# Merged input loads, four buffers of third weights and three of raw weights in the weight stage

## The chip, the cores and the metric

The kernel runs on one core of a Trainium2 chip. The metric is the time of the whole program on the device in microseconds, the median of the runs. A core has TensorE (PE in the profile), VectorE (DVE), ScalarE (ACT), GpSimd (POOL) and SyncE (SP); SP issues nearly all DMA transfers of this kernel.

## The reference, cut to what matters

```python
# attention with a decaying state, B, H, S, D = 4, 8, 768, 48
for t in range(S):
    cur = einsum('bhd,bhe->bhde', u[None] * kt, vt)
    y[:, :, t] = einsum('bhd,bhde->bhe', rt, state + cur)
    state = wt[:, :, :, None] * state + einsum('bhd,bhe->bhde', kt, vt)
# first feed-forward, x is y as [3072, 384], d_ff = 1024
h = ((x @ w1) * (x @ w2)) @ w3
x = h @ w_out
# second: gates choose two of 8 experts per token, then relu(x @ w1[e]) @ w2[e], weighted
```

## The kernel before

Attention goes batch by batch (4), and in a batch by pairs of heads (4). A pair is called g here, from 0 on, over all batches. One head of the pair lies on partitions 0 to 47, the other on 64 to 111. A pair needs the transposed w, k and r (tiles `wt`, `kt`, `rt`, [128, 768]), the rows of k and r (`kn`, `rn`) and of v (`vs`), each in two buffers by the parity of the pair.

The stage that this case is about is the first, some 106 us long. It threads two strands into one order, which every engine follows by itself (the list `order`):

- The attention of batch 0. For pair g the steps are "derive" (DVE: `dve_decays` L254, three reciprocals L265, `dve_keys` L272, `dve_queries` L278), "diag" (DVE: products L289 and L295, the sum L304), "spread" (ACT L317), "score" (PE L186, then the mask on DVE L325, in two halves), "keys" (PE transposes L195, ACT L245), "state" (PE L207, ACT L341, DVE L335), "scale" (ACT L353) and "out" (PE L231 and L237, ACT L360). The derive, diag and spread steps of pair g + 1 stand between the steps of pair g.
- The weights. `w_out` is turned and multiplied with the gates (L658, L667, L674), and then w3 @ w_out is built in eight blocks of rows, q = 0 to 7 ("w3_mm", four quarters each, PE L682). Block q reads `w3T[q % 2]`. ACT rounds the sum to `wah` (L598), and DVE takes the rest `wal` (L623). Beside it the six blocks of w1 and w2 come through `wraw` (two buffers) and are split into `w12h` (ACT L595, after the second quarter of blocks 1 to 6) and `w12l` (DVE L638).

Before its loop SP issues the loads of pairs 0 and 1, of w_out, of w3 blocks 0 and 1 (L526) and of raw blocks 0 and 1 (L532). In the loop, at the last quarter of block q, it asks for w3 block q + 2, once block q is done (`wa_full`), and for raw block q + 1, once `w12l_ready` has reached q. At the derive and diag steps of pair g it asks for the inputs of pair g + 2, at "out" it stores y and asks for v. The loads of pair 2 are the first that the loop issues, ahead of anything else.

`sp_input_load` loads w, k or r of a pair in two transfers, one for each head: 64 rows each for pairs 0 and 1 (which fills the pad rows once), 48 rows each from pair 2 on.

After this stage the feed-forward of batch b runs threaded with the attention of batch b + 1, then the experts. The first thing of it is L788 on PE, which needs the rounded y (`xh`, `xl`) of batch 0.

Of the kernel before, what the change touches and what calls it, by code (L numbers as in the profile page):

```python
# [7 lines left out]
F1 = 1024  # L8
E, F2 = 8, 1024
N = B * S  # L10
P = 128
# [21 lines left out]


TAIL = 3

WORDS = 16
PADS = 14
# [19 lines left out]
def program(nc, w_turned, k_turned, r_turned, k_rows, r_rows, v_rows, u, w1, w2, w3_turned, w_out, gate_rows, noise_rows, ew1, ew2_rows, out):  # L58
# [10 lines left out]
    with top:  # L69
# [70 lines left out]

        def sp_input_load(sp, b, q, n):
            g, i = HP * b + q, q % 2
            rows = HB if g < 2 else D
            need(sp, (decay_ready, kdiv_ready, rdec_ready)[n], g - 1)
            for h in range(2):
                sp.dma_start((wt, kt, rt)[n][i][h * HB:h * HB + rows, :],
                             (w_turned, k_turned, r_turned)[n][bass.ds(b, 1), 2 * q + h, 0:rows, :].rearrange("o d t -> (o d) t")
                             ).then_inc(loaded[n][i], 16)

        def sp_rows_load(sp, b, q):  # L150
            g, i = HP * b + q, q % 2
# [96 lines left out]
        def dve_decays(dve, b, q):  # L248

            g = HP * b + q  # L250
            dve.wait_ge(loaded[0][q % 2], 32 * (2 * b + q // 2 + 1))
            need(dve, state_ready, (NC - 1) * (g - 1))
            for c in range(NC):
                last = nc.vector.tensor_tensor_scan(decay[q % 2][:, c, 1:C + 1], wt[q % 2][:, c * C:(c + 1) * C],  # L254
                                                    wt[q % 2][:, c * C:(c + 1) * C], 1.0, ALU.mult, ALU.bypass)
            last.then_inc(decay_ready, 1)
# [10 lines left out]

        def dve_keys(dve, b, q):
            g = HP * b + q
            dve.wait_ge(loaded[1][q % 2], 32 * (2 * b + q // 2 + 1))  # L270
            dve.wait_ge(inverse_ready, 3 * (g + 1))
            nc.vector.tensor_tensor(kdiv[q % 2][:, :], kt[q % 2][:, :], kdiv[q % 2][:, :], ALU.mult).then_inc(kdiv_ready, 1)  # L272

        def dve_queries(dve, b, q):
            g = HP * b + q
            dve.wait_ge(loaded[2][q % 2], 32 * (2 * b + q // 2 + 1))
# [220 lines left out]

        with ExitStack() as ph:
            psb, psem = tools(ph)
            wraw = [psb(f"wraw{i}", [P, F1]) for i in range(2)]  # L500
            wo = psb("wo", [P, KF, WA])
            gates = psb("gates", [P, KD, 4 * E])
            woT = nc.alloc_sbuf_tensor_at("woT", [P, KD, F1], f32, offset=token_base)
            gates_side = nc.alloc_sbuf_tensor_at("gates_side", [P, 2 * P], f32, offset=token_base + 4 * KD * F1)
            w3T = [psb(f"w3T{i}", [P, KF, P]) for i in range(2)]
            pads = psb("pads", [P, PADS, WORDS], i32)
            wraw_loaded = [sem(f"wraw_loaded{i}") for i in range(2)]
            w12h_ready, w12l_ready = sem("w12h_ready"), sem("w12l_ready")
            wo_loaded, gates_loaded, w3_loaded = [sem(f"wo_loaded{i}") for i in range(2)], sem("gates_loaded"), [sem(f"w3_loaded{i}") for i in range(2)]
# [12 lines left out]

            def first_sp(sp):
                def load_w3(n):
                    need(sp, wa_full, n - 1)
                    sp.dma_start(w3T[n % 2][:, :, :].rearrange("p m j -> p (m j)"), w3_turned[n, :, :]).then_inc(w3_loaded[n % 2], 16)  # L526

                def load_w12(n):
                    m, kk = divmod(n, KD)
                    if n >= 2:  # L530
                        sp.wait_ge(w12l_ready, n - 1)
                    sp.dma_start(wraw[n % 2][:, :], (w1, w2)[m][kk * P:(kk + 1) * P, :]).then_inc(wraw_loaded[n % 2], 16)  # L532
# [12 lines left out]
                sp_values_load(sp, 0, 0)  # L545
                load_w3(1)
                for n in range(3):
                    sp_input_load(sp, 0, 1, n)
                sp_rows_load(sp, 0, 1)
                load_w12(0)  # L550
                sp_values_load(sp, 0, 1)
                load_w12(1)
                for step, q, n in order:
                    if step == "w3_mm" and n == 3:
                        if q + 2 < KF:
                            load_w3(q + 2)
                        if 1 <= q < 2 * KD - 1:
                            load_w12(q + 1)
                    elif step == "derive" or step == "diag":
                        sp_attention(sp, 0, step, q, n)  # L560
                    elif step == "out":
                        sp_attention(sp, 0, step, q, n)
                        if (q, n) == (1, 0):
                            sp.wait_ge(pads_ready, 1)
                            sp.dma_start(slot_entry.rearrange("(p a n) o -> p a (n o)", p=P, a=PADS),
                                         pads[:, :, :].rearrange("p n o -> p (n o)").rearrange("p (a x) -> p a x", a=1)
                                         .broadcast_to([P, PADS, PADS * WORDS])).then_inc(pads_stored, 16)
                            sp.wait_ge(zeros_ready, 1)
                            sp.dma_start(x2[N:N + 1, :].rearrange("o (h d) -> o h d", h=2),
                                         zeros[0:1, :].rearrange("p (h d) -> p h d", h=1).broadcast_to([1, 2, DM // 2])).then_inc(row_cleared, 16)  # L570
                        if (q, n) == (HP - 1, 1):
                            sp_group_load(sp, 0, 0, 1)
                    elif (step, q, n) == ("score", HP - 1, 1):
                        sp_group_load(sp, 0, 0, 0)

            def first_act(act):
# [7 lines left out]
                for step, q, n in order:  # L584
# [3 lines left out]
                    elif step == "wo_gates":  # L588
                        act.wait_ge(gates_full, 1)
                        nc.scalar.copy(gates_side[:, :], fx[:, 0:2 * P]).then_inc(gates_out, 1)  # L590
                    elif step == "w3_mm" and n == 1 and 1 <= q <= 2 * KD:

                        m, kk = divmod(q - 1, KD)
                        act.wait_ge(wraw_loaded[(q - 1) % 2], 16 * ((q - 1) // 2 + 1))
                        nc.scalar.copy(w12h[:, m, kk, :], wraw[(q - 1) % 2][:, :]).then_inc(w12h_ready, 1)  # L595
# [20 lines left out]
            def first_dve(dve):  # L616
# [10 lines left out]
                for step, q, n in order:  # L627
# [6 lines left out]
                    elif step == "w3_mm" and n == 2 and 1 <= q <= 2 * KD:  # L634

                        m, kk = divmod(q - 1, KD)
                        dve.wait_ge(w12h_ready, q)
                        nc.vector.tensor_tensor(w12l[:, m, kk, :], wraw[(q - 1) % 2][:, :], w12h[:, m, kk, :].bitcast(f32),  # L638
                                                ALU.subtract).then_inc(w12l_ready, 1)
                    elif step == "w3_mm" and n == 0 and q:  # L640
                        low(q - 1)
# [4 lines left out]
            def first_pe(pe):  # L646
                pe.wait_ge(ident_ready, 1)
                pe.wait_ge(pad_zero, 2)
                for step, q, n in order:
# [25 lines left out]
                        last.then_inc(gates_full, 1)  # L675
                    elif step == "w3_mm":
                        if n == 0:
                            pe.wait_ge(w3_loaded[q % 2], 16 * (q // 2 + 1))
                            pe.wait_ge(wo_ready, 1)
                            need(pe, wal_ready, q - 1)  # L680
                        for m in range(2 * n, 2 * n + 2):
                            last = nc.tensor.matmul(sums[q % 2][:, 0:WA], w3T[q % 2][:, m, :], wo[:, m, :],  # L682
                                                    start=(m == 0), stop=(m == KF - 1))
                        if n == 3:
                            last.then_inc(wa_full, 1)
# [998 lines left out]
def laid_out(np, inputs):  # L1684
# [1 line left out]
    a = {name: np.asarray(x) for name, x in inputs.items()}  # L1686

    def turned(x, fill):
        return np.pad(x.transpose(0, 1, 3, 2), [(0, 0), (0, 0), (0, HB - D), (0, 0)], constant_values=fill)

    def rows(x, pad):
        x = x.reshape(B, HP, 2, NC, P, D).transpose(0, 1, 4, 3, 2, 5)
# [30 lines left out]
```

## Time and profile before

| | us |
|---|---|
| median of 3 runs | 997.93 (997.01 to 1000.2) |
| the profiled execution, its time | 993.22 |
| its span, first to last instruction | 991.5 |
| PE busy in the span | 951.2 (96%) |
| DVE busy | 676.3 (68%) |
| ACT busy | 528.1 (53%) |

The profiled execution was 4.7 us shorter than the median of the runs; 1.7 us of its time lie outside the span. The span is that of one core, so there is no other core to wait for.

### The profile page before, as it was taken

What the parts mean: (1) busy time and instruction counts of PE and PEld (TensorE: products, weight loads), DVE (VectorE), ACT (ScalarE), POOL (GpSimd) and SP (SyncE); (2) the same over time, 40 slices, a digit from 0 to 9 for tenths busy, and PEclk for the clock granted to TensorE, in tenths of its full rate; (3) what the DMA queues carried; (4) which work ended last, traced back from release to release, by engine and by line L of the source; (5) the groups of instructions that cost most, each with busy time, mean ns of one, the idle gap of its engine ahead of it and who ended that gap; (6) DMA issues with size and microseconds to landing.
All of it is one profiled execution on the core that took longest, in us unless ns stands there. A gap on an engine that the chain in (4) does not pass through costs nothing.

```text
span 991.5 us, 18086 instructions
## 1 busy us (share of the span) xinstructions
PE 951.2 (96%) x6825; PEld 895.8 (90%) x6825; DVE 676.3 (68%) x1133; ACT 528.1 (53%) x986; POOL 221.3 (22%) x209
## 2 busy tenths in 40 slices
PE   5799999999999999999989999999999999999995
PEld 3455899999999999999989999999999999999995
DVE  5688886969696966256766685656856558566570
ACT  3354454555454645325644575655756557565560
POOL 0000000020202020221443323344232432324311
PEclk9889999999999999999999999999999999999998
DMA  9968434353435121216548797877968779787751
GB/s 262 295 190 263 142 85 143 105 160 95 143 106 172 57 71 41 81 52 217 177 123 244 196 294 214 241 257 205 308 206 243 262 202 301 211 245 258 212 152 17
DMA packets 93771, 179.61 MB, mean 181 GB/s; under 512 B 19042, under 2 KB 50532, under 8 KB 93684
## 3 DMA queue, kind: packets, MB, share of 16 engines
q1 hardware_dynamic: 80308, 157.77, 50.7%
q0 software_dynamic: 12976, 20.66, 10.1%
q8 instruction: 54, 0.88, 0.4%
q14 instruction: 33, 0.27, 0.1%
q10 hardware_dynamic: 400, 0.02, 0.0%
HBM read 152.81 MB, written 26.97 MB: 181 GB/s over the span
## 4 chain that ended last, share of the span: by engine, by line
PE 86%; DVE 3%; DMA 3%; ACT 2%; SPq 2%; issue 2%; another core or an unknown queue 0%; POOL 0%; DVEq 0%; ACTq 0%; POOLq 0%
PE pp L1233 20%; PE bank L1217 19%; PE bank L788 13%; PE bank L805 7%; PE fx L788 6%; PE fx L805 4%; PE yu L1276 3%; PE pp L186 2%; DMA w3T<-in_moe_w 2%; PE tr L1198 2%; PE yu L1258 1%; PE fx L1258 1%; PE yu L207 1%; PE yu L237 1%; DMA rn<-in_r_rows 1%
## 5 line engine op out<-in xcount | busy, mean ns | idle before, releaser
L1127 POOL DMA_INDIRECT result<-x2s,who x55 | 92.4, 1681 | 292.5 <-ACT x2s L1350 279.6
L1337 DVE SCALAR_TENSOR_TENSOR abl<-bank,abh 128x512 fp32r<-128x512 f32 x96 | 66.2, 691 | 113.7 <-ACT abh L1332 90.0
L978 POOL DMA_INDIRECT slot_entry<-entry,slot_i x48 | 52.1, 1086 | 334.6 <-DVE token_f L967 322.4
L1217 PE MATMUL bank<-xh,set_up_h 128*128 128x256 f32 x384 | 109.2, 284 | 0.0
L1217 PE MATMUL bank<-xh,set_up_l 128*128 128x256 f32 x384 | 108.6, 283 | 0.0
L1217 PE MATMUL bank<-xl,set_up_h 128*128 128x256 f32 x384 | 108.6, 283 | 0.0
L1332 ACT ACTIVATE abh<-bank 128x512 fp32r<-128x512 f32 x96 | 57.5, 599 | 85.1 <-PE bank L1217 80.2
L788 PE MATMUL bank<-xh,w12h 128*128 128x384 f32 x264 | 89.5, 339 | 1.0 <-DVE xl L485 0.9
L788 PE MATMUL bank<-xh,w12l 128*128 128x384 f32 x264 | 88.4, 335 | 0.0
L788 PE MATMUL bank<-xl,w12h 128*128 128x384 f32 x264 | 88.2, 334 | 0.0
L1233 PE MATMUL pp<-set_down_h,abh 128*128 128x384 f32 x256 | 87.7, 342 | 0.0
L1233 PE MATMUL pp<-set_down_h,abl 128*128 128x384 f32 x256 | 85.7, 335 | 0.0
L1233 PE MATMUL pp<-set_down_l,abh 128*128 128x384 f32 x256 | 85.6, 334 | 0.0
L265 DVE RECIPROCAL kdiv<-decay 128x256 f32<-128x256 f32 x48 | 82.2, 1734 | 0.3
L1114 POOL DMA_INDIRECT tokens<-ffn_out,who x55 | 72.6, 1319 | 32.9 <-issue 23.3
L1217 PEld LDWEIGHTS bank<-xh,set_up_h 128*128 128x128 f32 x384 | 73.5, 191 | 0.5 <-DVE abl L1337 0.2
L1217 PEld LDWEIGHTS bank<-xl,set_up_h 128*128 128x128 f32 x384 | 73.5, 192 | 0.3
L1217 PEld LDWEIGHTS bank<-xh,set_up_l 128*128 128x128 f32 x384 | 73.5, 191 | 0.0
L1350 ACT ACTIVATE x2s<-pp,who 128x384 f32<-128x384 f32 x48 | 28.0, 582 | 84.3 <-PE pp L1233 75.5
L317 ACT ACTIVATE att<-ident,diag 128x128 f32<-128x128 f32 x192 | 59.4, 389 | 15.0 <-DVE diag L304 15.0
L1305 DVE TENSOR_TENSOR set_up_l<-up_raw,set_up_h 128x1024 fp32r<-128x1024 f32 x48 | 57.6, 1224 | 9.3 <-ACT set_up_h L1300 8.8
L1305 DVE TENSOR_TENSOR w12l<-up_raw,w12h 128x1024 fp32r<-128x1024 f32 x45 | 55.0, 1223 | 8.5 <-ACT w12h L1300 5.6
(254 smaller groups left out, 2646.2 us busy)
## 6 DMA issues: line engine op xcount, KB each, us to landing
up_raw<-in_moe_w SPq DMA_DIRECT2D x93, 512.0 KB
down_raw<-in_moe_w SPq DMA_DIRECT2D x124, 384.0 KB
vs<-in_v_rows SPq DMA_DIRECT2D x16, 384.0 KB, 3.6
kn<-in_k_rows SPq DMA_DIRECT2D x16, 288.0 KB, 3.6
rn<-in_r_rows SPq DMA_DIRECT2D x16, 288.0 KB, 4.8
attention_out<-yt SPq DMA_DIRECT2D x64, 72.0 KB, 2.0
result<-zeros SPq DMA_DIRECT2D x12, 384.0 KB
ffn_out<-x2s SPq DMA_DIRECT2D x8, 576.0 KB
```

Of the source, the lines that this page charges most:

```text
L265: nc.vector.reciprocal(kdiv[q % 2][:, :].rearrange("p (c x) -> p c x", c=NC)[:, two, :], decay[q % 2][:, two, 1:C + 1]).then_inc(inverse_r ...
L317: last = nc.scalar.activation(att[:, j, h, c, :], ident[:, :], ACT.Copy, scale=diag[:, 3 * j + c, h:h + 1])
L788: last = nc.tensor.matmul(half_bank[n % 3][:, 0:TG], wp[:, m, kk, f * P:(f + 1) * P], xp[:, kk, :], start=(p == 0), stop=(p == 3 * KD - 1))
L805: last = nc.tensor.matmul(sum_at[s][:, 0:WA], xp[:, f, s * P:(s + 1) * P], wp[:, f, :], start=(f == 0 and n == 0), stop=(f == KF - 1 and n ...
L978: nc.gpsimd.indirect_dma_start(slot_entry, bass.IndirectOffsetOnAxis(slot_i[:, s, n:n + 1], 0), entry[:, s, n, :], None).then_inc(scattere ...
L1114: nc.gpsimd.indirect_dma_start(xg[v % 2][:, s, :], None, stored, bass.IndirectOffsetOnAxis(who[v % 4][:, s, 0:1], 0)).then_inc(gathered[v ...
L1127: nc.gpsimd.indirect_dma_start(out, bass.IndirectOffsetOnAxis(who[v % 4][:, s, 0:1], 0), yo[v % 2][:, s, 0:DM], None, bounds_check=N - 1, ...
L1217: last = nc.tensor.matmul(bank[m % 2][:, f * T2:(f + 1) * T2], wp[:, kk, c:c + P], xp[:, kk, :], start=(n == 0), stop=(n == 3 * KD - 1))
L1233: last = nc.tensor.matmul(pp[:, s, 0:DM], xp[:, f, s * P:(s + 1) * P], wp[:, f, :], start=(f == 0 and n == 0), stop=(f == KF - 1 and n == 2))
L1305: nc.vector.tensor_tensor(low, src, high.bitcast(f32), ALU.subtract).then_inc(w_low, 1)
L1332: nc.scalar.activation(hh[:, 2 * m:2 * m + 2, :].rearrange("p a t -> p (a t)"), bank[m % 2][:, :], ACT.Relu).then_inc(hh_ready, 1)
L1337: nc.vector.scalar_tensor_tensor(hl[:, 2 * m:2 * m + 2, :].rearrange("p a t -> p (a t)"), bank[m % 2][:, :], 0.0, hh[:, 2 * m:2 * m + 2, : ...
```

## The change

Two edits. (1) The arrays w, k and r are laid out in memory as [B, 4, 128, S], the two heads of a pair behind each other with the pad rows in them, so that one transfer of 128 partitions (384 KB) takes the place of two of 64 or 48 (192 or 144 KB each); the waits count 16 instead of 32. (2) `w3T` has four buffers instead of two, `wraw` three instead of two. Before the loop w3 blocks 2 and 3 and raw block 2 are asked for too; in the loop block q + 4 and raw block q + 2. What each of these loads waits for in the loop is unchanged (block q done; `w12l_ready` at q), it only fetches a later block.

```diff
+DEEP, RAW = 4, 3
         def sp_input_load(sp, b, q, n):
-            rows = HB if g < 2 else D
             need(sp, (decay_ready, kdiv_ready, rdec_ready)[n], g - 1)
-            for h in range(2):
-                sp.dma_start((wt, kt, rt)[n][i][h * HB:h * HB + rows, :],
-                             (w_turned, k_turned, r_turned)[n][bass.ds(b, 1), 2 * q + h, 0:rows, :].rearrange("o d t -> (o d) t")
-                             ).then_inc(loaded[n][i], 16)
+            sp.dma_start((wt, kt, rt)[n][i][:, :],
+                         (w_turned, k_turned, r_turned)[n][bass.ds(b, 1), q, :, :].rearrange("o x t -> (o x) t")
+                         ).then_inc(loaded[n][i], 16)
...
-            wraw = [psb(f"wraw{i}", [P, F1]) for i in range(2)]
+            wraw = [psb(f"wraw{i}", [P, F1]) for i in range(RAW)]
-            w3T = [psb(f"w3T{i}", [P, KF, P]) for i in range(2)]
+            w3T = [psb(f"w3T{i}", [P, KF, P]) for i in range(DEEP)]
...
                 def load_w3(n):
-                    need(sp, wa_full, n - 1)
+                    need(sp, wa_full, n - DEEP + 1)
...
                 def load_w12(n):
-                    if n >= 2:
-                        sp.wait_ge(w12l_ready, n - 1)
+                    need(sp, w12l_ready, n - RAW + 1)
...
                 load_w12(0)
                 sp_values_load(sp, 0, 1)
+                load_w3(2)
                 load_w12(1)
+                load_w3(3)
+                load_w12(2)
                 for step, q, n in order:
                     if step == "w3_mm" and n == 3:
-                        if q + 2 < KF:
-                            load_w3(q + 2)
-                        if 1 <= q < 2 * KD - 1:
-                            load_w12(q + 1)
+                        if q + DEEP < KF:
+                            load_w3(q + DEEP)
+                        if 1 <= q <= 2 * KD - RAW:
+                            load_w12(q + RAW - 1)
```

## Rows read from the trace of the kernel before

**Rows 1.** Page, part 2, granted TensorE clock in 40 equal slices.

```profile
...
PEclk9889999999999999999999999999999999999998
...
```

**Rows 2.** Busy time by stretch; last the clock, the DMA share and GB/s.

```profile
...
core 0: us, PE busy (x) PEld busy (x) DVE busy (x) ACT busy (x) POOL busy (x), PEclk, DMA share, GB/s
0.00:49.50 49.50, 30.32 (x198) 18.87 (x200) 29.14 (x43) 18.36 (x45) 1.72 (x13) 0.93 1.00 279
...
60.00:92.00 32.00, 28.66 (x201) 17.53 (x199) 27.90 (x41) 18.49 (x48) 0.00 (x0) 1.00 0.94 287
...
106.00:360.00 254.00, 254.00 (x2046) 239.71 (x2048) 205.50 (x420) 127.41 (x336) 26.12 (x24) 1.00 0.41 121
...
```

**Rows 3.** Timeline of PE: start, duration; idle time before it in brackets.

```profile
...
46.31 3.04 PE L682 MATMUL fx<-wo,w3T 128*128 128x400 f32 x4 [6.05 <-DMA w3T<-in_moe_w]
49.28 1.66 PE L186 MATMUL pp<-rdec,kdiv 48*128 48x128 f32 x12
50.86 1.31 PE L207 MATMUL yu<-vs,kend_t 128*64 128x48 f32 x20
...
59.15 1.61 PE L682 MATMUL fx<-wo,w3T 128*128 128x400 f32 x4
...
65.42 0.94 PE L186 MATMUL pp<-rdec,kdiv 48*128 48x128 f32 x12 [0.63 <-issue]
...
69.20 0.79 PE L207 MATMUL yu<-vs,kend_t 128*64 128x48 f32 x20
71.34 2.95 PE L682 MATMUL fx<-wo,w3T 128*128 128x400 f32 x8 [1.36 <-DMA w3T<-in_moe_w]
...
80.80 4.30 PE L682 MATMUL bank<-wo,w3T 128*128 128x400 f32 x12 [1.35 <-DMA w3T<-in_moe_w]
85.03 0.94 PE L186 MATMUL pp<-rdec,kdiv 48*128 48x128 f32 x12
...
```

**Rows 4.** Busy time by stretch around the longest wait.

```profile
...
42.00:46.00 4.00, 0.00 (x0) 0.00 (x0) 0.00 (x0) 0.00 (x0) 0.00 (x0) 0.54 1.05 251
...
50.00:56.00 6.00, 6.00 (x36) 3.97 (x33) 4.26 (x12) 2.84 (x7) 0.00 (x0) 0.50 0.05 20
56.00:60.00 4.00, 4.00 (x50) 2.68 (x49) 4.00 (x4) 0.96 (x2) 0.00 (x0) 1.00 0.25 74
...
```

**Rows 5.** Timeline of DVE, the same columns.

```profile
...
40.58 0.74 DVE L289 TENSOR_TENSOR ruk<-kn,rn 128x576 f32<-128x576 f32 x1
41.24 0.57 DVE L623 TENSOR_TENSOR wal<-bank,wah 128x400 fp32r<-128x400 f32 x1
51.05 1.01 DVE L325 COPY_PREDICATED att<-causal,pp 128x768 f32<-128x768 int32 x1 [9.24 <-PE pp L186]
...
53.70 2.00 DVE L254 TENSOR_TENSOR_SCAN decay<-wt 128x128 f32<-128x128 f32 x6
...
82.66 0.95 DVE L278 TENSOR_TENSOR rdec<-rt,decay 128x768 f32<-128x768 f32 x1
...
86.08 1.02 DVE L325 COPY_PREDICATED att<-causal,pp 128x768 f32<-128x768 int32 x1 [1.28 <-PE pp L186]
...
```

**Rows 6.** The chain that ended the first stage: start, duration, what.

```profile
...
7.79 10.19 DMA rn<-in_r_rows
...
```

**Rows 7.** Stretches of the first 40 us; the last column is GB/s.

```profile
...
2.75:5.50 2.75, 0.00 (x0) 0.00 (x0) 0.01 (x1) 0.01 (x1) 0.00 (x0) 1.00 1.00 233
...
8.00:13.80 5.80, 4.07 (x18) 3.48 (x19) 4.50 (x3) 1.81 (x4) 0.00 (x0) 1.00 1.07 262
...
19.00:25.00 6.00, 4.60 (x45) 3.20 (x47) 3.12 (x5) 4.40 (x14) 0.00 (x0) 1.00 1.03 241
25.00:28.00 3.00, 3.00 (x25) 1.78 (x20) 2.46 (x9) 1.91 (x6) 0.00 (x0) 1.00 1.04 357
31.00:38.50 7.50, 6.53 (x20) 3.41 (x18) 7.36 (x9) 4.64 (x14) 0.00 (x0) 1.00 1.04 232
...
```

**Rows 8.** Tile rn, the transfer of pair 2, issued at 22.21.

```profile
...
DMA to landing us min/median/max: 17.2/17.2/17.2
...
```

More of the change, by code:

```diff
@@ L250, in dve_decays @@
             g = HP * b + q
-            dve.wait_ge(loaded[0][q % 2], 32 * (2 * b + q // 2 + 1))
+            dve.wait_ge(loaded[0][q % 2], 16 * (2 * b + q // 2 + 1))
             need(dve, state_ready, (NC - 1) * (g - 1))
@@ L269, in dve_keys @@
             g = HP * b + q
-            dve.wait_ge(loaded[1][q % 2], 32 * (2 * b + q // 2 + 1))
+            dve.wait_ge(loaded[1][q % 2], 16 * (2 * b + q // 2 + 1))
             dve.wait_ge(inverse_ready, 3 * (g + 1))
@@ L275, in dve_queries @@
             g = HP * b + q
-            dve.wait_ge(loaded[2][q % 2], 32 * (2 * b + q // 2 + 1))
+            dve.wait_ge(loaded[2][q % 2], 16 * (2 * b + q // 2 + 1))
             need(dve, yu_full, 3 * (g - 1))
@@ L504, in program @@
             gates_side = nc.alloc_sbuf_tensor_at("gates_side", [P, 2 * P], f32, offset=token_base + 4 * KD * F1)
-            w3T = [psb(f"w3T{i}", [P, KF, P]) for i in range(2)]
+            w3T = [psb(f"w3T{i}", [P, KF, P]) for i in range(DEEP)]
             pads = psb("pads", [P, PADS, WORDS], i32)
-            wraw_loaded = [sem(f"wraw_loaded{i}") for i in range(2)]
+            wraw_loaded = [sem(f"wraw_loaded{i}") for i in range(RAW)]
             w12h_ready, w12l_ready = sem("w12h_ready"), sem("w12l_ready")
-            wo_loaded, gates_loaded, w3_loaded = [sem(f"wo_loaded{i}") for i in range(2)], sem("gates_loaded"), [sem(f"w3_loaded{i}") for i in range(2)]
+            wo_loaded, gates_loaded, w3_loaded = [sem(f"wo_loaded{i}") for i in range(2)], sem("gates_loaded"), [sem(f"w3_loaded{i}") for i in range(DEEP)]
             pads_ready, pads_stored, zeros_ready, row_cleared = (sem(x) for x in ("pads_ready", "pads_stored", "zeros_ready", "row_cleared"))
@@ L524, in load_w3 @@
                 def load_w3(n):
-                    need(sp, wa_full, n - 1)
-                    sp.dma_start(w3T[n % 2][:, :, :].rearrange("p m j -> p (m j)"), w3_turned[n, :, :]).then_inc(w3_loaded[n % 2], 16)
+                    need(sp, wa_full, n - DEEP + 1)
+                    sp.dma_start(w3T[n % DEEP][:, :, :].rearrange("p m j -> p (m j)"), w3_turned[n, :, :]).then_inc(w3_loaded[n % DEEP], 16)
                 def load_w12(n):
                     m, kk = divmod(n, KD)
-                    if n >= 2:
-                        sp.wait_ge(w12l_ready, n - 1)
-                    sp.dma_start(wraw[n % 2][:, :], (w1, w2)[m][kk * P:(kk + 1) * P, :]).then_inc(wraw_loaded[n % 2], 16)
+                    need(sp, w12l_ready, n - RAW + 1)
+                    sp.dma_start(wraw[n % RAW][:, :], (w1, w2)[m][kk * P:(kk + 1) * P, :]).then_inc(wraw_loaded[n % RAW], 16)
                 sp_input_load(sp, 0, 0, 0)
@@ L593, in first_act @@
                         m, kk = divmod(q - 1, KD)
-                        act.wait_ge(wraw_loaded[(q - 1) % 2], 16 * ((q - 1) // 2 + 1))
-                        nc.scalar.copy(w12h[:, m, kk, :], wraw[(q - 1) % 2][:, :]).then_inc(w12h_ready, 1)
+                        act.wait_ge(wraw_loaded[(q - 1) % RAW], 16 * ((q - 1) // RAW + 1))
+                        nc.scalar.copy(w12h[:, m, kk, :], wraw[(q - 1) % RAW][:, :]).then_inc(w12h_ready, 1)
                     elif step == "w3_mm" and n == 3:
@@ L637, in first_dve @@
                         dve.wait_ge(w12h_ready, q)
-                        nc.vector.tensor_tensor(w12l[:, m, kk, :], wraw[(q - 1) % 2][:, :], w12h[:, m, kk, :].bitcast(f32),
+                        nc.vector.tensor_tensor(w12l[:, m, kk, :], wraw[(q - 1) % RAW][:, :], w12h[:, m, kk, :].bitcast(f32),
                                                 ALU.subtract).then_inc(w12l_ready, 1)
@@ L677, in first_pe @@
                         if n == 0:
-                            pe.wait_ge(w3_loaded[q % 2], 16 * (q // 2 + 1))
+                            pe.wait_ge(w3_loaded[q % DEEP], 16 * (q // DEEP + 1))
                             pe.wait_ge(wo_ready, 1)
@@ L681, in first_pe @@
                         for m in range(2 * n, 2 * n + 2):
-                            last = nc.tensor.matmul(sums[q % 2][:, 0:WA], w3T[q % 2][:, m, :], wo[:, m, :],
+                            last = nc.tensor.matmul(sums[q % 2][:, 0:WA], w3T[q % DEEP][:, m, :], wo[:, m, :],
                                                     start=(m == 0), stop=(m == KF - 1))
@@ L1688, in turned @@
     def turned(x, fill):
-        return np.pad(x.transpose(0, 1, 3, 2), [(0, 0), (0, 0), (0, HB - D), (0, 0)], constant_values=fill)
+        x = np.pad(x.transpose(0, 1, 3, 2), [(0, 0), (0, 0), (0, HB - D), (0, 0)], constant_values=fill)
+        return x.reshape(B, HP, 2 * HB, S)
     def rows(x, pad):
```

## The prediction, made before the result was known

> **What bounds the kernel now.** I read the page's slices first, then the busy times by stretch, the waits of PE and its timeline, last DVE's. The clock line shows full clock but for a stretch in the first twentieth [rows 1]. From 106 us to 360 us PE is busy for all of its 254.00 us [rows 2]; later it is nearly so (waits of 5.4 us in all after 106 us, by the chain of waits). So what is won or lost in the first 106 us is carried to the end one for one, and nothing behind it can be won by a faster load. The attention inputs of batches 1 to 3 are loaded in those PE-bound stretches, at a DMA share of 0.41, and neither PE nor DVE waits for one there: merging them, and the 96 KB more in each, is priced at nothing, covered by PE's work. If that cover were gone, each would cost at most its landing, 2.4 to 3.1 us.
>
> In the first stage three things take turns. Up to 49.5 us the DMA engines are full (share 1.00, 279 GB/s) [rows 2]. At 40.26 us PE has done the scores and transposes of pair 1, finds w3 block 2 not there (SP asked for it at 35.99 us only, when block 0 was done and DVE's and ACT's results were stored), and waits 6.05 us [rows 3]. During that wait the granted clock falls to half (0.54, then 0.50) and is full again in the stretch from 56 us [rows 4], so that four matmuls take 3.04 us where they take 1.61, the second scores 1.66 where they take 0.94, the state products 1.31 for 0.79 [rows 3]. DVE sits idle for 9.24 us of that, waiting for these scores [rows 5]. From 53.70 us on DVE is all but full: 4.00 of 4.00 us and 27.90 of 32 [rows 2, 4]. PE waits for w3 twice more, 1.36 and 1.35 us [rows 3].
>
> **The change, part by part.**
>
> *w3 blocks 2 and 3 asked for ahead of the loop.* They are queued behind v of pair 1 and stand in the queue where raw block 1 stands now, which landed at 33.4 us (issued at 15.59, 17.8 us to landing): before 38 us, while PE wants block 2 at 40.3. The wait goes. What is late next? The mask at 51.05 us waits for the scores; these come earlier by the wait, 6.05, plus 3.04 - 1.61 = 1.43, plus 1.66 - 0.94 = 0.72: 8.2 us. The state products after them, at full clock, give another 0.4 (of 1.31 - 0.79 = 0.52) before DVE's next scan at 53.70. DVE could take the mask from 41.24 + 0.57 = 41.81 on, and now gets it at 51.05 - 8.2 = 42.85, so PE still decides. Sum here: 8.6 us, bounds 8.2 and 8.7.
>
> *From there to the end of the stage.* DVE is the bound until the queries of pair 2, and moves as one. PE then waits about 2.5 us for them instead of 0.63: it has its work moved by as much, and no w3 to wait for. Blocks 4 and 5 are in their own buffers long before, so 1.36 + 1.35 = 2.71 us of PE waits go. They count only as far as DVE lets them: the scores at 85.03 need the queries that DVE ends at 82.66 + 0.95 = 83.61, so 85.03 - 83.61 = 1.4 us count, and the mask's own wait of 1.28 closes [rows 3, 5]. From 85 us to the end of block 7 PE has no gap. Term: 1.4, bounds 0 and 1.4.
>
> *The third raw buffer.* Raw block 2 is asked for at 15 instead of 40 us. ACT waits 1.35 us for a raw block once, at 73.3 us, off the chain that counts. Nothing by itself. The issues: six transfers less before the loop, three more. SP's issues (0.4 to 1 us each) run far ahead of the full DMA engines. Nothing either.
>
> *Merged loads of pairs 0 and 1.* The same bytes (384 KB a tile). The stage's start hangs on r's rows of pair 0, issued at 7.79 and landing at 18.0 us [rows 6]. In the stretches in which w, k and r pass, the rate is low: 233 GB/s from 2.75 us, 262 from 8 us, 241 from 19 us, 232 from 31 us; where the 128-row tiles pass it is 357 [rows 7]. If that is from the half-tile shape, the first two stretches (0.64 + 1.52 = 2.16 MB in 8.55 us) take 6.05 us: 2.5 us less ahead of r's rows. If it is not, nothing is won. The Trainium skill has this as a rule (SBUF — State Buffer, "Door 1: The DMA port swizzle"): partitions 0 to 63 reach only 8 of the 16 ports, and two transfers to the two halves do not add up. The trace agrees in kind, 232 to 262 against 357 GB/s; by the rule alone the gain would be the 2.5 us. The rows cannot separate the shape from what else is in flight, so I take half: 1.3 us, bounds 0 and 2.5. PE's leg in this place has 1.7 us of slack and its w_out halves move with it.
>
> *What the early loads push back.* This speaks against the change. Three weight blocks, 1.57 MB, and 0.29 MB of new pad rows now stand ahead of the rows of k and r of pair 2, which landed at 22.2 + 17.2 = 39.4 us [rows 8]; DVE wants them at 40.58 [rows 5], and behind that product stand `wal` (0.57) and the mask of pair 1, on which state, output and all the rest of DVE hang. At 279 GB/s these 1.86 MB are 6.7 us: landing at 46.1. At the full rate the weights take 1.57 / 0.357 = 4.4 us, and the four slow stretches (5.35 MB in 22.05 us, 15.8 us with the pad rows at 357) give back 6.25: landing at 37.6. With half of that gain, 39.4 - 3.1 + 4.4 = 40.7 us. The product may start up to 41.2 - 1.3 = 39.9 us without holding the mask. So 0.8 us are lost, bounds 0 and 4.9 (ready at 46.1 + 0.7 + 0.5 = 47.3 against 42.45). The Trainium skill's rule (DMA: Bandwidth & Descriptors, "Queues, rings and completion order": each engine consumes its ring in order) is why I count all that is ahead; the landings here come in about that order.
>
> The other inputs of pair 2 (w wanted at some 44 us, k and r later) land before these rows. In the loop SP waits at the same places as before, so nothing new is queued behind a wait. The stage's later bytes are spread more evenly: after 49.5 us the DMA engines stood nearly still for ten.
>
> **Sum.** 8.6 + 1.4 + 1.3 - 0.8 = 10.5 us. The profiled execution took 993.22 us, so the same one would take 982.7. Its ratio, 0.9894, on the median of 997.93 gives 987.4 us.
>
> **The rivals.**
>
> *A: as summed, 9 to 12.5 us won.* Chance 0.55. High end: 8.7 + 1.4 + 2.5 = 12.6, 985.3 us.
>
> *B: pair 2's rows come late.* DVE's wait moves from the scores to this transfer and is 3 to 5 us long. No rate is won from merging: 8.6 + 1.4 - 4.9 = 5.1 us, about 993 us. For it: the same pair of w, k, r is also slow in a stretch with other tiles in it, 31 to 38.5 us. Against it: 357 and more where they are absent. Chance 0.27 for 4 to 9 us.
>
> *C: the clock falls again.* PE now waits for DVE at the outputs and queries of pairs 1 and 2, 2 to 3 us each. Waits of up to 1.4 us left the clock full, one of 6.05 did not; between them the trace shows nothing. Repeating the old loss costs 1.43 + 0.72 + 0.4, and eight to sixteen slow matmuls that PE has partly the slack for: 2.5 to 5 us off, so 991 us. Chance 0.08.
>
> *D: no change that shows (within 0.3%, 3 us, which is about what a measurement here tells from nothing).* B and C together: 5.1 - 2.5 = 2.6 us. Chance 0.06.
>
> *E: slower.* One mechanism: the rows of pair 2 land so late that the mask of pair 1 starts later than 51.05 us. That needs landing after 51.05 - 0.5 - 0.7 = 49.8, thus 10.4 us for 1.86 MB, or 179 GB/s, below every stretch of [rows 7]. At that point it gives 998 less the 1.4 of the later waits; at 54.5 us it is over 0.3% slower, 1001 us. Chance 0.04.
>
> **How the numbers follow.** Faster by over 0.3%: A, B, C, 0.90; same 0.06; slower 0.04. The likeliest is A at 987.4. The range: from A's high end, 985 us, to past B's 993, at 994 us; D, E and the edges are left out, some 0.15.
>
> **What would show it.** Right: no wait for w3 on PE behind the first block, and full clock from 40 to 56 us; the mask of pair 1 before 43 us; the scan behind it at 43 to 45 us; the rate from 8 to 25 us above 300 GB/s; r's rows of pair 0 before 17.2 us; the first L788 at 95 to 96 us instead of 105.97. Wrong: a wait of DVE at L289 for the rows of pair 2 of more than 2 us (B), a clock below 1 after a wait for DVE (C), or a first L788 moved as forecast with a span that is not (the later stages are then not carried one for one).

## The result and the profile after

| | before | changed |
|---|---|---|
| median | 997.47 us (993.61 to 1000.2, 4 runs) | 983.39 us (980.43 to 983.89, 4 runs) |
| the profiled execution | 993.22 us | 983.89 us |
| its span | 991.5 us | 982.1 us |

The ratio is 0.9855, 95% interval 0.9817 to 0.9894: 14.1 us less by the medians, at least some 10 us. 987.4 us with a range of 985.0 to 994.0 had been forecast, so the direction was right and the time lies 1.6 us below the range. One execution of the kernel with one early request took 1562.99 us at a granted clock of 0.562; it is left out of that kernel's numbers below.

The first view is the busy time by stretch of the changed kernel, in the stretches of [rows 7] and one more (last columns: clock, DMA share, GB/s):

```profile
core 0: us, PE busy (x) PEld busy (x) DVE busy (x) ACT busy (x) POOL busy (x), PEclk, DMA share, GB/s
2.75:5.50 2.75, 0.00 (x0) 0.00 (x0) 0.82 (x3) 0.01 (x1) 0.00 (x0) 1.00 1.05 358
8.00:13.80 5.80, 4.90 (x41) 3.44 (x43) 5.60 (x6) 3.41 (x6) 0.00 (x0) 1.00 0.89 340
19.00:25.00 6.00, 4.88 (x52) 3.19 (x56) 4.35 (x12) 3.92 (x12) 0.00 (x0) 1.00 1.04 406
...
31.00:38.50 7.50, 6.39 (x40) 3.86 (x40) 7.08 (x8) 5.51 (x15) 0.00 (x0) 1.00 1.06 398
...
72.00:76.00 4.00, 4.00 (x15) 2.44 (x15) 1.83 (x3) 0.89 (x2) 0.00 (x0) 0.58 0.71 237
```

From 2.75 us the rate is 358 GB/s where it was 233, from 8 us 340 for 262, from 19 us 406 for 241, from 31 us 398 for 232. The prediction's fullest rate was 357; half of the way to it had been assumed. The last row is a stretch in which the clock was at its lower level (1.2 of 2.4 GHz) for most of the time, which the kernel before did not have there.

PE's timeline of the changed kernel, first to last what answers to [rows 3] (start, duration, idle time before it in brackets):

```profile
36.49 1.51 PE L683 MATMUL fx<-wo,w3T 128*128 128x400 f32 x4
37.93 0.94 PE L185 MATMUL pp<-rdec,kdiv 48*128 48x128 f32 x12
38.79 0.79 PE L206 MATMUL yu<-vs,kend_t 128*64 128x48 f32 x20
...
52.84 0.94 PE L185 MATMUL pp<-rdec,kdiv 48*128 48x128 f32 x12 [2.54 <-DVE kdiv L271]
...
71.13 0.94 PE L185 MATMUL pp<-rdec,kdiv 48*128 48x128 f32 x12 [1.67 <-DVE kdiv L271]
72.00 1.33 PE L194 MATMUL tr<-ident,kdiv 128*128 128x128 f32 x5
73.12 2.64 PE L683 MATMUL bank<-wo,w3T 128*128 128x400 f32 x4
...
93.73 0.44 PE L789 MATMUL bank<-xh,w12h 128*128 128x384 f32 x1 [0.90 <-DVE xl L484]
```

w3 block 2 starts at 36.49 right behind the transposes, without a wait and at full clock: four matmuls in 1.51 us, scores 0.94, state 0.79. Nothing waits for w3 any more. PE's waits are now for DVE's keys and queries, 2.54 and 1.67 us. Behind the second of them the transposes take 1.33 us for 0.77, and four matmuls 2.64 for 1.51.

DVE's timeline of the changed kernel, for [rows 5]:

```profile
13.73 0.76 DVE L288 TENSOR_TENSOR ruk<-kn,rn 128x576 f32<-128x576 f32 x1
15.24 0.76 DVE L294 TENSOR_TENSOR ruk<-ruk,u_all 128x576 f32<-128x576 f32 x1 [0.76 <-DMA u_all<-in_u]
...
23.38 2.00 DVE L253 TENSOR_TENSOR_SCAN decay<-wt 128x128 f32<-128x128 f32 x6
...
36.98 0.73 DVE L288 TENSOR_TENSOR ruk<-kn,rn 128x576 f32<-128x576 f32 x1
...
38.98 1.02 DVE L324 COPY_PREDICATED att<-causal,pp 128x768 f32<-128x768 int32 x1 [0.78 <-PE pp L185]
...
41.12 2.00 DVE L253 TENSOR_TENSOR_SCAN decay<-wt 128x128 f32<-128x128 f32 x6
...
70.08 0.95 DVE L277 TENSOR_TENSOR rdec<-rt,decay 128x768 f32<-128x768 f32 x1
...
76.75 1.02 DVE L324 COPY_PREDICATED att<-causal,pp 128x768 f32<-128x768 int32 x1 [2.92 <-PE pp L185]
```

The rows of pair 0 are there at 13.7 us (asked for at 4.67, 9.0 us to landing), 4.3 us before their time; they are also asked for 3.1 us earlier than before, where it was 7.79 [rows 6]. Now `u_all` is last, with a wait of 0.76 us. The rows of pair 2 (issued at 20.70, 13.6 us to landing) are there at 34.3 us, before DVE wants them at 36.98: no wait. The mask of pair 1 starts at 38.98 instead of 51.05. The mask that starts at 76.75 has waited 2.92 us for PE's scores, over the half-clock stretch.

What counts is where the stage's marks stand, in us from the start (a table put together from the timelines of all kernels, which the next section explains; "scan" is L254 of before, "mask" the second half of pair 1, "group" the first matmul of the first feed-forward group):

| | scan, pair 1 | mask, pair 1 | scan, pair 2 | group | span |
|---|---|---|---|---|---|
| before | 27.01 | 51.05 | 53.70 | 105.97 | 991.5 |
| changed | 23.38 | 38.98 | 41.12 | 93.73 | 982.1 |
| before, second trace | 29.57 | 52.39 | 55.05 | 107.70 | 991.1 |
| changed, second trace | 23.40 | 39.00 | 41.14 | 92.08 | 975.9 |
| merging alone | 23.09 | 39.72 | 41.86 | 94.42 | 976.2 |
| early requests alone | 28.98 | 47.87 | 49.85 | 102.41 | 984.1 |
| changed, 64-row halves | 28.88 | 46.21 | 48.19 | 102.15 | 983.7 |
| changed, column halves | 24.64 | 40.75 | 42.89 | 95.46 | 977.7 |
| before, one early request | 28.90 | 45.56 | 47.54 | 101.56 | 983.2 |
| changed, third trace | 23.21 | 38.80 | 40.94 | 93.57 | 980.6 |
| changed, 2, 6, 4 fillers | 22.97 | 40.43 | 42.56 | 95.89 | 977.6 |
| changed, 1, 3, 2 fillers | 23.16 | 38.75 | 40.89 | 91.83 | 978.5 |
| changed, `u_all` by ACT | 24.30 | 39.89 | 42.03 | 94.60 | 979.7 |
| the same with 1, 3, 2 fillers | 24.43 | 40.95 | 43.08 | 94.02 | 977.8 |

In the first pair of traces the group moved by 12.24 us and the span by 9.4. The 2.8 us between were lost behind the stage: up to the group at 405 us of before the distance is 12.24 us, at 430 it is 11.0 (PE waited 0.94 us for an ACT copy of the sums that had been free before), at 470 10.8, at 504 10.75, and from 526 on 9.16. In that last part the changed kernel's clock was 0.66 over 5 us where the other's was 1.00. The second pair of traces, taken on one chip, shows 15.6 us at the group, still 15.6 at 620 us, and 15.2 in the span.

### The profile page after: what moved, and what is told of

The parts are those of the page before. It is cut to its first block, busy times and chain, and to the rows that moved or that the text cites. A ratio compares the mean times of both kernels' runs of the same rounds, so it can differ in the third digit from the quotient of the medians.

```text
span 982.1 us, 18038 instructions
## 1 busy us (share of the span) xinstructions
PE 947.8 (97%) x6825; PEld 894.9 (91%) x6825; DVE 676.3 (69%) x1133; ACT 527.6 (54%) x986; POOL 220.6 (22%) x209
## 4 chain that ended last, share of the span: by engine, by line
PE 86%; DVE 6%; ACT 3%; issue 3%; DMA 1%; another core or an unknown queue 1%; SPq 0%; POOL 0%; DVEq 0%; ACTq 0%; POOLq 0%
PE pp L1234 20%; PE bank L1218 20%; PE bank L789 13%; PE bank L806 7%; PE fx L789 6%; PE fx L806 4%; PE yu L1277 3%; PE pp L185 3%; PE tr L1199 2%; PE yu L1259 1%; PE fx L1259 1%; DVE kdiv L264 1%; PE yu L206 1%; PE tr L194 1%; DMA u_all<-in_u 1%
```

## The experiments

The kernels were timed in three sets of four, in the order below, each set on one chip and with the kernel before beside it. Ratios and differences of medians are against the kernel before of the same set.

**The two edits apart.** Merging alone, DEEP and RAW at 2:

```diff
-DEEP, RAW = 4, 3
+DEEP, RAW = 2, 2
...
-                load_w3(2)
                 load_w12(1)
-                load_w3(3)
-                load_w12(2)
```

> Merged input loads alone; w3T and wraw with two buffers as before, none of the early requests. Theory M (the merged transfers raised the rate of the whole front, so the queue is short when w3 block 2 is asked for): the first scan of pair 1 starts near 23.4 us as in the changed kernel, w3 block 2, asked for near 31 us, lands by 37 us, PE waits for it less than 1.5 us and the clock stays full there; first L789-type matmul (the first group's) at 94 to 97 us, time 9 to 14 us less than before. Theory D (the early requests carry it): the scan of pair 1 3.6 us earlier, but PE still waits 4 us or more for block 2 and the clock falls; first group's matmul at 100 to 103 us, time 3 to 6 us less than before.

Measured: 978.01 us, ratio 0.9878 (0.985 to 0.9907), 13.2 us less than the kernel before (991.24). PE's timeline:

```profile
37.12 1.61 PE L680 MATMUL fx<-wo,w3T 128*128 128x400 f32 x4 [0.77 <-DMA w3T<-in_moe_w]
...
94.42 0.44 PE L786 MATMUL bank<-xh,w12h 128*128 128x384 f32 x1 [0.90 <-DVE xl L484]
```

Block 2 is asked for at 30.86 us, still only when block 0 is done, and lands 6.2 us later instead of 10.3, at 37.06. PE waits 0.77 us, and the clock stays full behind it. Theory M holds, theory D does not: with full rate the queue is short when the block is asked for, and early requests are hardly needed. What they add on top is seen from the scan of pair 1 to that of pair 2: 18.77 us here, 17.74 in the changed kernel, so 1.0 us. By the time of the whole kernel (interval 0.985 to 0.9907 against 0.9817 to 0.9894, in different sets) that cannot be told from nothing.

Early requests alone, w, k and r in two transfers of 64 or 48 rows as before:

```diff
+            rows = HB if g < 2 else D
-            sp.dma_start((wt, kt, rt)[n][i][:, :], ...
+            for h in range(2):
+                sp.dma_start((wt, kt, rt)[n][i][h * HB:h * HB + rows, :], ...
```

> Four and three buffers with the early requests alone; w, k and r in two transfers of 64 or 48 rows as before. Theory M: no gain ahead of pair 1's scan (27.0 us as before), the rate from 19 to 38 us stays at 230 to 320 GB/s, the rows of pair 2 land at 44 to 46 us and DVE waits for them 3 to 5 us; mask of pair 1 at 45 to 47.5 us; first group's matmul at 99 to 101 us, 5 to 7 us less than before. Theory D: mask of pair 1 at 42 to 43 us, first group's matmul at 96 to 97 us, 9 to 10 us less.

Measured: 984.75 us, ratio 0.9938 (0.9919 to 0.9958), 6.5 us less. DVE's timeline:

```profile
28.98 2.00 DVE L255 TENSOR_TENSOR_SCAN decay<-wt 128x128 f32<-128x128 f32 x6
...
46.72 0.76 DVE L290 TENSOR_TENSOR ruk<-kn,rn 128x576 f32<-128x576 f32 x1 [4.04 <-DMA rn<-in_r_rows]
...
47.87 0.99 DVE L326 COPY_PREDICATED att<-causal,pp 128x768 f32<-128x768 int32 x1
```

Here is what the prediction's rival B described: DVE waits 4.04 us for the rows of pair 2, which stand behind the early weights in a slow queue, and the mask of pair 1 starts at 47.87. The first group was at 102.41 us, later than the 99 to 101 expected: the scan of pair 1 was at 28.98 instead of 27.0 (in the second trace of before it is at 29.57), and two half-clock stretches of 3.4 us fell into the stage, from 50.8 us and from 81.6 us.

**What makes the transfers slow.** The changed kernel with the same layout in memory and the same bytes, each tile cut by rows:

```diff
+            for h in range(2):
+                sp.dma_start((wt, kt, rt)[n][i][h * HB:(h + 1) * HB, :],
+                             (w_turned, k_turned, r_turned)[n][bass.ds(b, 1), q, h * HB:(h + 1) * HB, :].rearrange("o x t -> (o x) t")
+                             ).then_inc(loaded[n][i], 16)
```

> The changed kernel with each w, k and r tile in two transfers of 64 rows: the same bytes and the same layout in memory, other tiles as in the changed kernel. If the shape of 64 rows sets the rate (theory S): rates of 230 to 300 GB/s in the stretches 2.75 to 5.5, 8 to 13.8 and 19 to 25 us, scan of pair 1 at 26 to 27.5 us, first group's matmul at 98 to 102 us. If the layout in memory or anything else of the change set it (theory L): the same rates of 340 to 410 as the changed kernel, scan of pair 1 at 23.5 to 24, first group's matmul at 94 us.

and cut by columns, so that each transfer touches all 128 partitions:

```diff
+            for h in range(2):
+                sp.dma_start((wt, kt, rt)[n][i][:, h * TG:(h + 1) * TG],
+                             (w_turned, k_turned, r_turned)[n][bass.ds(b, 1), q, :, h * TG:(h + 1) * TG].rearrange("o x t -> (o x) t")
+                             ).then_inc(loaded[n][i], 16)
```

> The changed kernel with each w, k and r tile in two transfers of 128 rows and half of the columns (192 KB, rows of 1536 bytes). As many transfers as with 64 rows, but each over all partitions. Theory S (rows of the half tile): as the changed kernel, rates of 340 to 410, scan of pair 1 at 23.4 to 24.5, first group's matmul at 93.5 to 95. If the number of transfers or of issues sets it (theory N): scan of pair 1 at 26 to 27.5, first group's matmul at 98 to 102.

Measured: 986.46 us, ratio 0.9964 (0.994 to 0.9987), for the row halves; 979.61 us, ratio 0.9893 (0.9855 to 0.9931), for the column halves. Busy time by stretch of the row halves, then of the column halves:

```profile
2.75:5.50 2.75, 0.00 (x0) 0.00 (x0) 0.22 (x1) 0.02 (x1) 0.00 (x0) 1.00 0.91 211
...
19.00:25.00 6.00, 5.51 (x26) 3.77 (x23) 3.22 (x5) 4.26 (x14) 0.00 (x0) 1.00 1.05 244
```

```profile
2.75:5.50 2.75, 0.00 (x0) 0.00 (x0) 1.45 (x5) 0.02 (x1) 0.00 (x0) 1.00 0.92 284
...
19.00:25.00 6.00, 4.59 (x39) 2.60 (x38) 3.38 (x8) 5.08 (x17) 0.00 (x0) 0.86 1.05 403
```

244 GB/s from 19 us by rows, 403 by columns, with equal bytes and equally many transfers. Theory S holds in the main: the transfers over 64 partitions are what is slow. The Trainium skill (SBUF — State Buffer, "Door 1: The DMA port swizzle") has the rule, that partitions 0 to 63 reach 8 of the 16 ports; an estimate from it gives a single such stream half of the rate, and the trace agrees in kind, with 244 against 403 GB/s in the mix with whole tiles; no run here has such a stream alone. Halves by columns are not free either: 284 GB/s for 358 in the first stretch, and DVE waits for the rows of pair 0:

```profile
15.26 0.76 DVE L289 TENSOR_TENSOR ruk<-kn,rn 128x576 f32<-128x576 f32 x1 [1.87 <-DMA rn<-in_r_rows]
```

The scan of pair 1 comes 1.3 us later than with one transfer (24.64 against 23.38), with row halves 5.5 us later (28.88); both are somewhat later than theory S had them (24.5 at most, and 27.5). The 1.3 us point at theory N in small. SP's timeline of the column halves, and below it that of the changed kernel, has the request for r's rows:

```profile
6.96 0.44 SPq L154 DMA_DIRECT2D rn<-in_r_rows  x1
```

```profile
4.67 0.43 SPq L153 DMA_DIRECT2D rn<-in_r_rows  x1
```

With twice as many transfers for w, k and r the rows are asked for 2.3 us later, and in the first 5.5 us the DMA share is 0.59 instead of 0.68. In the set of these runs the scan of pair 1 stood at 28.88 us with row halves, 24.64 with column halves and 23.09 with merging alone: 4.2 us for the shape and 1.6 us for what is left between two transfers and one. That these 1.6 us are the later requests alone was not shown, since the column halves also have rows half as long in memory.

**Both kernels once more, on one chip.** No edit.

> The kernel before once more, for its trace on the same chip as the three others: scan of pair 1 at 27 to 29 us, PE's wait for w3 block 2 of 5 to 7 us, half clock behind it, first group's matmul at 105 to 108 us. If the wait of 6 us was an accident of the first trace (rival), it is under 3 us here and the first group's matmul at 100 us.

> The changed kernel once more, with its time taken in five rounds. Theory: scan of pair 1 at 23.4, first group's matmul at 92 to 94 us; a half-clock stretch of 2 to 4 us behind one of PE's waits for DVE (2.5 or 1.7 us) appears again, though not always behind the same one; 12 to 14 us less than before. If the half-clock stretch of the first trace was an accident, none here and the first group's matmul at 92.1 us.

Measured: the kernel before 992.78 us in the one execution with the trace; the changed one 977.65 us, ratio 0.9851 (0.9818 to 0.9885), 15.0 us less than the median of before (992.66). PE's timeline of the kernel before, and below it DVE's scan of pair 1:

```profile
47.66 3.04 PE L682 MATMUL fx<-wo,w3T 128*128 128x400 f32 x4 [4.83 <-DMA w3T<-in_moe_w]
...
107.70 0.58 PE L788 MATMUL bank<-xh,w12h 128*128 128x384 f32 x1 [0.90 <-DVE xl L485]
```

```profile
29.57 2.00 DVE L254 TENSOR_TENSOR_SCAN decay<-wt 128x128 f32<-128x128 f32 x6
```

The wait for block 2 is no accident, 4.83 us here, a little under the 5 to 7 expected. The front moves by 2.6 us between two traces of the same kernel (27.01 and 29.57), while that of the changed kernel does not (23.38 and 23.40). PE's timeline of the changed kernel, and the stretch at the start of the first group:

```profile
52.85 0.94 PE L185 MATMUL pp<-rdec,kdiv 48*128 48x128 f32 x12 [2.53 <-DVE kdiv L271]
...
71.14 0.94 PE L185 MATMUL pp<-rdec,kdiv 48*128 48x128 f32 x12 [1.67 <-DVE kdiv L271]
...
92.08 0.50 PE L789 MATMUL bank<-xh,w12h 128*128 128x384 f32 x1 [0.90 <-DVE xl L484]
```

```profile
92.00:96.00 4.00, 3.92 (x13) 3.92 (x14) 1.59 (x3) 0.48 (x1) 0.00 (x0) 0.57 0.62 203
```

With waits of 2.53 and 1.67 us as in the first trace, the stage itself kept its full clock, and the group stands at 92.08, 1.65 us earlier than in the first trace. The half-clock stretch (0.57) came right behind, at the group's start, which had waited 0.90 us. The second trace of before has one there too (0.50 from 108 to 110 us). The expectation, one stretch again and not always at the same place, holds.

**Early requests without merging, priced by the prediction's sum.** The kernel before, with w3 block 2 alone ahead of the loop:

```diff
+DEEP = 3
-            w3T = [psb(f"w3T{i}", [P, KF, P]) for i in range(2)]
+            w3T = [psb(f"w3T{i}", [P, KF, P]) for i in range(DEEP)]
...
                 sp_values_load(sp, 0, 1)
+                load_w3(2)
                 load_w12(1)
...
-                        if q + 2 < KF:
-                            load_w3(q + 2)
+                        if q + DEEP < KF:
+                            load_w3(q + DEEP)
```

> The kernel before with three w3 buffers and w3 block 2 alone requested ahead of the loop (0.52 MB); input loads in half tiles, two raw buffers. The sum of the prediction without merging: the wait and the clock behind it give 8.6 us, the rows of pair 2 come 1.5 to 2.3 us later (41 to 42 us on the first trace's clock), so DVE waits for them under 1.5 us; first group's matmul 8 to 10 us before that of the kernel before in the same call, 7 to 10 us less time. Rival (half tiles keep the queue so long that something else is late): 3 to 6 us.

Measured: 982.58 us (five executions), ratio 0.9894 (0.9855 to 0.9933), 10.1 us less. DVE's timeline, then PE's:

```profile
44.40 0.76 DVE L290 TENSOR_TENSOR ruk<-kn,rn 128x576 f32<-128x576 f32 x1 [1.80 <-DMA rn<-in_r_rows]
...
66.29 1.02 DVE L326 COPY_PREDICATED att<-causal,pp 128x768 f32<-128x768 int32 x1 [3.63 <-PE pp L187]
```

```profile
59.25 1.65 PE L187 MATMUL pp<-rdec,kdiv 48*128 48x128 f32 x12 [3.21 <-DVE kdiv L273]
```

DVE waits 1.80 us for the rows of pair 2, a little over what was expected; the first group comes 6.1 us earlier than in the second trace of before, on the same chip (101.56 against 107.70), not 8 to 10. The missing part is seen at 59.25: PE had waited 3.21 us for DVE and went on at half clock (scores 1.65 us for 0.94), and a mask waited 3.63 us. The time, 10.1 us less, is better than the stage shows. 1.6 us more come right behind it, where the kernel before has its half-clock stretch at the group and this one has none: from 112.60 us on the distance of the two traces is 7.71 us, and the spans are 7.9 us apart (991.1 and 983.2). The profiled execution was the slowest of the five (984.96 us), 2.4 us above their median, which is the size of the rest. One early block of 0.52 MB won more than three weight blocks of 1.57 MB (0.9894 against 0.9938, in different sets): with half tiles the pushback is real.

**The clock behind PE's waits.** First fillers: matmuls of `ident` with `wo` into an idle PSUM bank, read by nobody.

```diff
                 for step, q, n in order:
+                    if step == "score" and n == 0:
+                        for _ in range((0, 2, 6, 4)[q]):
+                            nc.tensor.matmul(bank[0][:, 0:WA], ident[:, :], wo[:, 0, :], start=True, stop=True)
                     pe_attention(pe, 0, step, q, n)
```

> The changed kernel with 2, 6 and 4 matmuls of 400 columns, whose result nobody reads, ahead of the first scores of pairs 1, 2 and 3, where PE waited 1.1, 2.5 and 1.7 us for DVE. If the waits bring the clock down (rival C of the prediction in small): full clock through the whole first stage, the mask of 2.92 us wait at 76.8 waits 1.3 us only, first group's matmul at 91.5 to 92.5 us, 1 to 2 us less than the changed kernel. If the fall has another cause: it stays, first group's matmul at 93.5 to 95 us and the same time or more.

Measured: 978.04 us, ratio 0.9855 (0.9821 to 0.9888), no better than the changed kernel in that set (977.65). PE's timeline, the two fillers of pair 1:

```profile
35.03 1.51 PE L653 MATMUL bank<-wo,ident 128*128 128x400 f32 x4
```

Two matmuls are four rows and take 1.51 us: I had counted a row for a matmul and filled twice the wait. Each first mask waited 0.95 to 1.84 us for it, and the group came at 95.89 us. Behind the filled waits the clock stayed full, but it fell at a place without a filler, to half from 21.4 to 24.8 us, behind a wait of 1.07 us that ended at 19.36 with the mask of pair 0. The expectation of full clock through the stage was missed. As a price it says little, and it was done again with 1, 3 and 2, beside the changed kernel on the same chip:

```diff
-                        for _ in range((0, 2, 6, 4)[q]):
+                        for _ in range((0, 1, 3, 2)[q]):
```

> The changed kernel, to compare with the three others of this call. As before: scan of pair 1 at 23.4 us, first group's matmul at 92 to 94 us (92.1 where no half-clock stretch falls into the stage, 93.7 where one does).

> The changed kernel with 1, 3 and 2 filler matmuls ahead of the first scores of pairs 1, 2 and 3 (0.72 us each as measured, so 0.7, 2.2 and 1.4 us in waits of 1.1, 2.5 and 1.7). If the waits bring the clock down: full clock through the stage in each profile, first group's matmul at 92.1 us, and full clock behind it too; time as the changed kernel or up to 2 us less. If the half-clock stretches have another cause: one of 2 to 4 us in or just behind the stage as in the changed kernel's traces.

Measured: 981.70 us (981.01 to 982.34), ratio 0.9852 (0.9817 to 0.9886), for the changed kernel; 979.90 us (977.80 to 980.28), ratio 0.9829 (0.9802 to 0.9856), with the fillers. No run of the one overlaps a run of the other; the difference is 1.8 us. PE's timeline with fillers (L653 are the fillers), and the busy time of the stage with them and, below, without:

```profile
49.91 2.18 PE L653 MATMUL bank<-wo,ident 128*128 128x400 f32 x6
...
69.06 1.51 PE L653 MATMUL bank<-wo,ident 128*128 128x400 f32 x4
...
91.83 0.44 PE L792 MATMUL bank<-xh,w12h 128*128 128x384 f32 x1 [0.91 <-DVE xl L484]
```

```profile
0.00:97.00 97.00, 85.17 (x630) 55.40 (x631) 81.35 (x118) 48.98 (x123) 4.16 (x51) 1.00 0.84 291
```

```profile
0.00:97.00 97.00, 80.56 (x587) 51.92 (x587) 80.02 (x116) 48.80 (x122) 4.14 (x51) 0.98 0.82 288
```

The fillers end before the scores start, the clock is 1.00 over the whole 97 us of this trace instead of 0.98, and the group is at 91.83 us instead of 93.57 in the same set's trace without them: 1.74 us, the size of the measured difference. This version has the lowest ratio of all, though its interval overlaps those of the changed kernel.

How far this shows the cause is seen from all traces together. Without fillers the clock fell behind the wait of 2.5 us in two of the six traces with merged or column-halved loads (merging alone, `u_all` by ACT) and behind that of 1.7 us in three (changed, first and third trace, column halves); in one it fell behind neither. In the three traces with fillers it never fell behind either. That supports that PE's waits let it fall, but what picks the wait is open: two of the three traces with fillers had their half-clock stretch at about 22 us instead, behind a wait of 1.06 us which no filler covered and which left the clock full in the other traces, the column halves excepted.

**The new last one in the front.** `u_all` issued by ACT ahead, and that with the fillers:

```diff
+                nc.scalar.dma_start(u_all[:, :, :, :].rearrange("p q h d -> p (q h d)"),
+                                    bass.AP(u.tensor, u.offset, [[0, P], [1, H * D]])).then_inc(small_loaded, 16)
```

> The changed kernel with u (192 KB) issued by ScalarE behind the gates, at about 1.5 us, instead of by SyncE behind the rows of pair 0, at 5.1 us. DVE waited 0.76 us for it, and the chain of the stage hung on it. If that wait is all of it: no wait at the second product, scan of pair 1 at 22.6 us, first group's matmul 0.8 us earlier (91.3 or 92.9 us), time 0 to 1.5 us less. If u, now ahead of w_out, pushes w_out and the rows back by its own 192 KB (0.5 us) or more: scan of pair 1 at 23.1 to 23.9, no gain.

> Both: u by ScalarE and the 1, 3 and 2 filler matmuls. Best case the sum of both: first group's matmul at 91.3 us, full clock in the stage, time 1 to 3 us less than the changed kernel. If neither tells: within 1 us of it.

Measured: 984.00 us, ratio 0.9885 (0.9857 to 0.9912), and with the fillers 980.91 us, ratio 0.9849 (0.9819 to 0.9878). DVE's timeline of the first of the two:

```profile
15.35 0.76 DVE L288 TENSOR_TENSOR ruk<-kn,rn 128x576 f32<-128x576 f32 x1 [1.85 <-DMA rn<-in_r_rows]
```

The wait for `u_all` is gone, and one of 1.85 us for the rows of pair 0 has taken its place; w_out comes later too. The scan of pair 1 is at 24.30 us, 0.9 to 1.1 later than with u in its old place: the unfavourable expectation, and slightly worse than it. The time is 2.3 us more than the changed kernel's. Both together are 0.8 us better than the changed kernel and 1.0 us worse than the fillers alone; against `u_all` by ACT without fillers, the fillers win 3.1 us. The group of both together is at 94.02 us, far from the 91.3 expected: the front is as late as with `u_all` by ACT alone (scan of pair 1 at 24.43), and the clock fell at 22.3 us, ahead of the first filler. The view of that stretch:

```profile
19.00:25.00 6.00, 4.59 (x38) 2.77 (x37) 3.59 (x8) 4.75 (x15) 0.00 (x0) 0.78 1.04 405
```

## Why the prediction was off

**The step that failed** is the term "Merged loads of pairs 0 and 1": 1.3 us, bounds 0 and 2.5. It measured 3.63 us in the first pair of traces and 6.17 on one chip (scan of pair 1: 27.01 to 23.38, 29.57 to 23.40). Row and column halves show that the shape of the transfer was the greater part of its cause (4.2 of 5.8 us in their set), the case of which I had taken half. The upper bound was wrong as well. The rate itself did what the bound said: 358 and 340 GB/s in the two stretches ahead of r's rows for the 357 assumed, some 2.3 of the 2.5 us. But the bound let the same bytes pass ahead of these rows. Up to and with them the tiles hold 3.87 MB; before, some 4.8 MB had been moved by their landing at 18.0 us (224 GB/s over 10 us, 317 over the next 8), in the changed kernel 4.1 MB (296 GB/s over 13.7 us). These 0.7 MB of transfers issued later are another 2 us, an estimate at the 358 GB/s of the front. It is open why they moved beside the rows. It isn't the half tiles alone: with column halves 4.5 MB had been moved (297 GB/s over 15.2 us), with row halves 4.7 MB (253 over 18.6). A term put at nothing belongs here too: SP's issues were said to run far ahead of full DMA engines, but r's rows were asked for at 7.79 us and are now at 4.67, and the step from two transfers to one was worth up to 1.6 us at the scan.

**The wait for w3 and the half clock behind it**, 8.6 us: 12.58 - 3.63 = 8.95 us from scan to scan in the first pair of traces, 13.91 - 6.17 = 7.74 in the second, where the wait had been 4.83 instead of 6.05. The mechanism was right, and the size nearly (bounds 8.2 and 8.7). But the attribution was not: it was put down to the early requests, and merging alone gives all but 1.0 us of it. Each of the two edits does away with this wait by itself, so their gains (13.2 and 6.5 us in one set) are more together than the 14 to 15 us of both.

**What the early loads push back**, -0.8 us: nothing. The rows of pair 2 landed at 34.3 us, 2.7 us ahead of need; even the favourable landing, 37.6 us, was 3.3 us too late. Here the rate was too low: 357 GB/s was the best stretch of the old mix, and it is 406 and 398 from 19 and 31 us without half tiles. With half tiles the wait is there: 4.04 us with three blocks, 1.80 with one, between the bounds of 0 and 4.9. So rival B is what the early requests do by themselves.

**To the end of the stage**, 1.4 us: mask and group moved by another 1.7 us in the trace without a half-clock stretch in the stage (13.91 to 15.62), a little over the upper bound of 1.4. In the first trace it was taken away again: 12.58 at the scan, 13.9 at the scores of pair 3, 12.24 at the group. Rival C, a fall of the clock behind waits of 2.5 us, had 0.08 and a price of 2.5 to 5 us. The fall is real, at about 1.7 us a time in the changed kernel, and came in nearly every trace in some place; not as a case of its own, but on top of A.

**The loads of batches 1 to 3 and the third raw buffer** cost nothing that shows: PE was busy for 254.00 of 254 us before, and in the changed kernel nothing waits for w, k or r there. "Carried to the end one for one" held on one chip (15.6 and 15.2 us) and only in part in the first pair (12.2 and 9.4), where waits and a half-clock stretch between 405 and 526 us took 2.8 us.

The sum with the measured terms is 3.63 + 8.95 + 1.32 - 1.66 = 12.24 us for the first pair, 6.17 + 7.74 + 1.71 = 15.62 us for the second, where 10.5 had been forecast. The three timings of the changed kernel, with ratios of 0.9855, 0.9851 and 0.9852, have medians 14.1, 15.0 and 13.5 us below those of the kernel before.

## What to carry to other kernels

Look at the rate in the stretches of a full queue before asking where a request stands in it: if it depends on which tiles pass, their shape comes first, and every early request gets cheaper by it. Here a transfer over all 128 partitions with padding beat two over the halves with less data. Two edits that remove the same wait don't add; price each with the other already done. And when a wait of PE is replaced by a shorter one for another engine, the clock behind it is part of the price; useless matmuls sized to the wait won 1.8 us here, but the clock can fall behind another wait instead.

## What was not expected of the hardware

- Whole tiles came at 397 to 408 GB/s over the stretches of 6 and 7.5 us from 19 and 31 us, in three traces of the changed kernel; no stretch of the first trace of before that was looked at in its first 40 us had more than 382.
- The front of the kernel before differs between two traces (scan of pair 1 at 27.0 and 29.6 us), that of the changed one hardly (23.4, 23.4, 23.2).
- `u_all`, 192 KB broadcast from one row of 1.5 KB, took 10.0 us from issue to landing, behind the rows. Issued first, it held up the rows of pair 0 by more than its bytes, which at 358 GB/s would be an estimated 0.5 us: they landed 2.0 us later than in the same set's trace of the changed kernel (15.3 and 13.3 us), and DVE waited 1.85 us for them where it had not waited.
- Half-clock stretches of some 3 to 4 us follow waits of PE of only 0.9 to 2.5 us, not always behind the same one, and cost 1.65 to 1.75 us each in this stage. At waits of 3.21 us (row halves, one early request) the stretch lasted nearly 7 us.
